# Two second-layer groups of each expert moved behind the next expert's first two first-layer groups

## The reference, cut to what matters

```
logits = x @ w_gate ; expert = argmax(logits) ; gate = softmax(logits)[expert]
for each token in order: it takes the next slot of its expert (at most 384 slots per expert)
h = relu(einsum('ecd,edf->ecf', disp, w1))        # 384 -> 1024, for each expert
y = einsum('ecf,efd->ecd', h, w2)                 # 1024 -> 384
out[token] = gate * y[expert, slot]
```

## Time and profile before

| what | value |
|---|---|
| median of 3 runs | 415.98 us (415.86 to 416.11) |
| span of the profiled execution, first to last instruction | 413.8 us |
| TensorE matmul busy | 406.2 us, 98% of the span |
| VectorE, ScalarE, GpSimd busy | 243.7, 188.1, 231.0 us |
| granted TensorE clock | full in all slices, mean 0.999 |

### The profile page before, as it was taken

How to read it: one execution, slowest core, us unless ns; L and a number is a source line. 1 busy time by engine, 2 the same in 40 slices (tenths; PEclk the granted TensorE clock), 3 DMA queues, 4 the chain that set the end, 5 groups by cost and what they waited for, 6 DMA issues and landing times.

```text
span 413.8 us, 9451 instructions
## 1 busy us (share of the span) xinstructions
PE 406.2 (98%) x3697; PEld 390.8 (94%) x3697; DVE 243.7 (59%) x576; ACT 188.1 (45%) x409; POOL 231.0 (56%) x239
## 2 busy tenths in 40 slices
PE   8999999999999999999999999999999999999994
PEld 8799799999999999999999999999999999999994
DVE  7787955376576547654653487785635556364521
ACT  4786543233433333333343555553645445464420
POOL 3789775467856685668234336075073461825531
PEclk9999999999999999999999999999999999999999
DMA  7998996204030403020018001827383845729000
GB/s 287 402 396 351 367 344 243 82 38 148 12 119 2 139 21 118 3 86 21 2 20 344 2 2 38 326 77 248 125 308 101 340 160 203 295 89 360 5 31 28
DMA packets 18650, 64.98 MB, mean 157 GB/s; under 512 B 2203, under 2 KB 11717, under 8 KB 16432
## 3 DMA queue, kind: packets, MB, share of 16 engines
q1 hardware_dynamic: 16672, 59.67, 39.5%
q0 software_dynamic: 1792, 4.73, 3.0%
q10 hardware_dynamic: 144, 0.00, 0.0%
HBM read 51.98 MB, written 13.21 MB: 158 GB/s over the span
## 4 chain that ended last, share of the span: by engine, by line
PE 92%; DVE 4%; issue 1%; POOL 1%; ACT 1%; DMA 0%; POOLq 0%; DVEq 0%
PE bank L1362 27%; PE bank L1364 26%; PE bank L1363 26%; PE bank L1383 2%; PE bank L1412 1%; PE bank L1448 1%; PE bank L1452 1%; PE bank L1686 1%; PE bank L1441 1%; PE bank L1444 1%; PE bank L1539 1%; PE bank L1721 1%; PE bank L1722 1%; PE bank L1725 1%; PE bank L1625 1%
## 5 line engine op out<-in xcount | busy, mean ns | idle before, releaser
L707 POOL TENSOR_TENSOR g_lo<-elu,g_hi 128x256 fp32r<-128x256 f32 x95 | 73.8, 778 | 86.5 <-ACT g_hi L875 86.3
L1362 PE MATMUL bank<-xt,wd_hi 128*128 128x256 f32 x285 | 80.7, 283 | 0.6 <-DVE elu L1190 0.6
L1364 PE MATMUL bank<-xt,wd_lo 128*128 128x256 f32 x285 | 80.5, 282 | 0.0
L1363 PE MATMUL bank<-xt,wd_hi 128*128 128x256 f32 x285 | 80.4, 282 | 0.0
L866 ACT ACTIVATE elu<-elu 128x256 f32<-128x256 f32 x96 | 40.1, 418 | 76.5 <-DVE elu L1182 75.9
L1362 PE MATMUL bank<-wd_hi,g_hi 128*128 128x392 f32 (+1 forms) x192 | 67.5, 352 | 0.0
L1364 PE MATMUL bank<-wd_hi,g_lo 128*128 128x392 f32 (+1 forms) x192 | 65.3, 340 | 0.0
L1363 PE MATMUL bank<-wd_lo,g_hi 128*128 128x392 f32 (+1 forms) x192 | 65.2, 339 | 0.0
L1190 DVE SCALAR_TENSOR_TENSOR elu<-elu,bank 128x256 f32<-128x256 f32 x96 | 40.3, 420 | 40.5 <-ACT elu L866 40.5
L875 ACT CAST g_hi<-elu 128x256 fp32r<-128x256 f32 x96 | 39.0, 406 | 45.0 <-DVE elu L1190 45.0
L1362 PEld LDWEIGHTS bank<-xt,wd_hi 128*128 128x128 f32 x285 | 54.0, 189 | 1.3 <-DVE elu L1190 1.1
(11 more groups left out here) (220 smaller groups left out, 946.2 us busy)
## 6 DMA issues: line engine op xcount, KB each, us to landing
we_raw<-wexp SPq DMA_DIRECT2D x8, 1536.0 KB, 6.5
wd_raw<-wexp SPq DMA_DIRECT2D x8, 1536.0 KB, 7.7
rkt<-rkt SPq DMA_DIRECT2D x12, 512.0 KB, 5.5
nat<-nat SPq DMA_DIRECT2D x9, 672.0 KB, 5.0
xrow<-slots SPq DMA_DIRECT2D x16, 193.0 KB, 7.3
wd_raw<-win SPq DMA_DIRECT2D x4, 768.0 KB, 8.0
wd_raw<-wout SPq DMA_DIRECT2D x4, 768.0 KB, 8.9
wo_tr<-wouttr SPq DMA_DIRECT2D x1, 3072.0 KB, 17.8
```

The source lines that it names most:

```text
L707: nc.gpsimd.tensor_tensor(g_lo[:, f % 4, :], elu[:, f % 2, :], g_hi[:, f % 4, :].bitcast(F32), ALU.subtract).then_inc(s_glo, 1)
L1362: mm(dst, w_hi, x_hi, start=start, stop=False)
L1363: mm(dst, w_hi, x_lo, start=False, stop=False)
L1364: return mm(dst, w_lo, x_hi, start=False, stop=stop)
```

## The change

`expert` on TensorE no longer ends with fc2(6) and fc2(7). They are issued in the next expert, fc2(6) behind its fc1(0) and fc2(7) behind its fc1(1). fc2(0) of the next expert follows fc1(2) as before. Expert 1 has nothing behind it (`behind` false, since expert 0 has another form), and expert 7 still issues all of its own. The two gate multiplications of an expert move on VectorE to behind `ge_lo` of group 1 of the next expert. Two waits are split or loosened: fc1(0) waits for one `ge_lo` less, and fc2(0) waits for the `yrow` of each tile apart. Waits on the other engines' and SyncE's side are as before.

```diff
 # VectorE
+            def expert_out(i, r):
+                for t in range(2):
+                    if t == 0:
+                        dve.wait_ge(s_y0, 2 * i + r + 1)
+                    else:
+                        dve.wait_ge(s_fc2e, ET * (2 * i + r + 1))
+                    V.tensor_scalar(yrow[r][:, t, :], ps_ye[t][:, 0:DM], xrow[r][:, t, GATE:GATE + 1], None,
+                                    ALU.mult).then_inc(s_ye[r], 1)
-            def expert(i, r, more):
+            def expert(i, r, more, behind):
                 ni, nr = (i, 1) if r == 0 else (i + 1, 0)
+                bi, br = (i - 1, 1) if r == 0 else (i, 0)
                 for f in range(ET):
...
+                    if f == 1 and behind:
+                        expert_out(bi, br)
...
+                if not more:
+                    expert_out(i, r)
 # TensorE, fc2_expert
-                    y_before, n_before = other(s_ye, r, i)
-                    wait_if(pe, y_before, 2 * n_before)
                 for t in tiles:
+                    if f == 0:
+                        y_before, n_before = other(s_ye, r, i)
+                        pe.wait_ge(y_before, 2 * n_before - 1 + t)
 # TensorE, expert
-                    wait_if(pe, s_gelo, q if f == 0 else q - 1)
+                    wait_if(pe, s_gelo, q - 1)
...
                     last.then_inc(s_he, 1)
+                    if f < 2 and behind:
+                        fc2_expert(bi, br, ET - 2 + f)
                     if more and f >= 2:
                         fc2_expert(i, r, f - 2)
...
-                if more:
-                    fc2_expert(i, r, ET - 2)
-                    fc2_expert(i, r, ET - 1)
-                else:
+                if not more:
 # both engines
-            expert(0, 1, True)
+            expert(0, 1, True, False)
...
-                expert(i, 0, True)
-                expert(i, 1, True)
-            expert(NE // 2 - 1, 0, True)
-            expert(NE // 2 - 1, 1, False)
+                expert(i, 0, True, True)
+                expert(i, 1, True, True)
+            expert(NE // 2 - 1, 0, True, True)
+            expert(NE // 2 - 1, 1, False, True)
```

More of the change, by code:

```diff
@@ L1308, in expert @@
                         V.tensor_copy(tok_i[r][:, :, :], xrow[r][:, :, TOKEN:XR]).then_inc(s_tok[r], 1)
-                for t in range(2):
-                    if t == 0:
-                        dve.wait_ge(s_y0, 2 * i + r + 1)
-                    else:
-                        dve.wait_ge(s_fc2e, ET * (2 * i + r + 1))
-                    V.tensor_scalar(yrow[r][:, t, :], ps_ye[t][:, 0:DM], xrow[r][:, t, GATE:GATE + 1], None,
-                                    ALU.mult).then_inc(s_ye[r], 1)
+                if not more:
+                    expert_out(i, r)
             tile_row(s_he, ET, s_lrow)
```

## The result

The changed kernel takes 418.35 us (median of 5 runs, 418.03 to 419.11), the kernel before 415.86 beside it: ratio 1.0069, 95% interval 1.0058 to 1.008. That is 0.7% slower, 2.5 us. The value lies inside the stated range, but it isn't the forecast of 416.0: it is where rival 1 (the loads are late in full, 418.3 to 419.7, chance 0.36) put it. The profiled execution has a span of 417.0 us, 3.2 above the one before; at 418.82 us it was one of the longer of the five.

What follows compares the result with a forecast made beforehand. TensorE, busy 98% of the span, was taken as the bound. From 415.98 us, -0.94 for the removed gap and +1.0 for late rows gave 416.0 us, own range 415.2 to 416.8; full range 414.9 to 419.2.

Steps and rivals of the forecast that it cites:

- rival 1: SyncE's loads late in full, no overlap of fetch and pause helping: net +2.4 to +3.7, 418.3 to 419.7 us, chance 0.36.
- The gain: TensorE at fc1(2): the wait for fc1(0)'s bank goes in six of seven places, 6 x 0.156 = 0.94 us.
- The place of the loss: SyncE's queue: W2 issued 5.21 and rows 6.1 us behind W1, transposes waiting for late rows, 1.0 us (0.2 to 1.7).
- The `yrow` multiplications: VectorE's two gate multiplications, moved behind `ge_lo`: both tiles ready for fc2(0) in time by 0.4 us, cost nothing.
- the signs of being wrong: In the changed profile: transposes idle 1 us and more, or none; fc2(0)'s weight load idle; fetches not 5 to 7 us behind W1.
- So the rows land 0.9 to 1.4 us later.: SyncE's row loads behind W2: landing shift; experts 5 and 6 in time or late by 0.1, before any fetch effect.
- the pause of W2 issued alone: DMA engines after a lone W2 issue: full flow only 2.3 us behind it, 1.4 us of flow lost.
- a fetch there costs the loads much less: Instruction fetches of experts 3, 4, 7 fall where little flows, 5.6 to 7.5 us behind W1: rows late by 0 to 0.5.
- the 415.0: Time if W2 loads at the skill's price, landing 0.5 us earlier: no row late, sum -0.94.
- GpSimd's 0.11 us: fc2(0)'s wait for W2's three low parts: margin falls from 0.27 to 0.11 us ahead of the weight load, should just hold.
- rival 3: At fc2(0), the gap only moved to a wait for GpSimd or `yrow`: net 0 on its own, counted inside the forecast's 0.40.
- Nothing there: GpSimd's scatter of `yrow`, queued behind the W2 pieces until 306.23: `yrow` at 305.95 still ahead, so no cost.

Runs made afterwards that it cites:

- both waits out of the way: Changed kernel with row loads issued ahead of W1 and fc2(0), fc2(2), fc2(5) each waiting only for its GpSimd W2 piece: 414.75 us; old order with early rows 415.79.
- experiment 4: Changed kernel, but fc2(0), fc2(2) and fc2(5) wait for GpSimd's first, second and third W2 piece: 418.65 us, ratio 1.0065.
- the half move: Against the changed kernel, fc2(6) stays in its expert, only fc2(7) goes behind the next fc1(0), gate multiplications behind `ge_lo` of group 0: 421.8 us, ratio 1.0157.
- experiment 1: Kernel before, TensorE's order untouched, SyncE holding W2 of experts 3 to 7 until the next expert's fc1(1): 418.04 us, ratio 1.0051.
- the kernels with the rows ahead of W1: Gates copied aside on VectorE, row loads issued before W1: changed kernel 415.48 us, kernel before 415.79; with finer W2 waits, full change 414.75, fc2(7) alone moved 414.69.
- experiment 3: Changed kernel with SyncE's last two loads exchanged, rows first, then W2: 417.89 us, ratio 1.0044.

## Why the prediction was right and wrong

**What held.** The gain: the gap at fc1(2) is gone in six places, and with both waits out of the way the move gives about 1.0 us (415.79 to 414.75), against 0.94. The place of the loss: W2 and rows out at 5.2 and 6.1, the transposes late, all five. The `yrow` multiplications are in time (nothing at fc2(0) is left once GpSimd's wait is finer). VectorE's other work cost nothing.

**How much of that is luck.** The range holds 418.35 because it was drawn round the rivals too. The forecast's own 416.0, with 415.2 to 416.8, missed it by 2.35 us, and a slower kernel had a chance of 0.36 only. The time lies at the lower end of rival 1. Two of the signs of being wrong that the prediction names did show: idle of 1 us and more at the transposes (1.03 and 1.32), and a late weight load at fc2(0).

**What failed.** The forecast fell on one step: "So the rows land 0.9 to 1.4 us later." For experts 5 and 6, whose loads had no instruction fetch of 0.02 MB in them, it was 2.1 and 2.0, and TensorE idled 0.85 and 0.34 us for them instead of 0 to 0.1. The other three places, which the forecast built on these two, idled 3.0 us together instead of 0.9. I took the pause of W2 issued alone and let everything behind it run at the old rate. The windows show that the rate itself falls, to 266 GB/s over 6 us, and that the pause is the smaller part of it. The term was 1.4 us at most, and measured 1.9 to 2.1. The lower bound of 0.9 rests on a W2 that lands 6.1 us behind its issue, as a W1 does, though the row of the W2 issued alone says 8.0; measured were 6.4 to 7.5.

**The fetch.** Experts 3, 4 and 7, with a fetch among their packets, were shifted by 1.1, 0.6 and 1.0 us only, so the difference between them and 5 and 6 fell from about 1.6 us to 0.4. That is what the step "a fetch there costs the loads much less" said. It is consistent with it and not shown: no run was made to move a fetch. In one run of experiment 4 (the finer wait alone) expert 7's fetch lay 0.9 us behind W1 instead of 5.1, and its rows landed at 14.1 instead of 14.5; expert 3's, with the fetch where it was, differ more between the same two runs (14.2 and 15.1), so this doesn't decide it. Rival 1 got the time right for a partly wrong reason: its price rested on three late places with 5 and 6 in time; measured were five late ones, each by about 0.3 to 1.3.

**The price of a transfer.** W2 took 6.4 to 7.5 us when issued at 5.24 in the changed kernel and 8.6 to 9.8 at 4.18 in the half move. The Trainium skill, in DMA: Bandwidth & Descriptors (Anatomy of one DMA), fits a transfer issued by GpSimd with 2.0 us and the rest at 436 GB/s, which would be an estimate of 5.6 us. These loads are issued by SyncE, for which that section gives no fit, and no W2 here was that fast, so the 415.0 that would follow from it didn't come.

**GpSimd's 0.11 us** of margin did not hold. I had taken 0.04 us for the semaphore, from a VectorE row; from GpSimd's end (324.67) to the weight load (324.91) it is 0.24. That is rival 3, 0.3 to 0.4 us, counted inside the forecast. In the changed kernel it cost nothing that can be told (418.35 us with it, 418.65 with the finer wait), because the late rows come behind it.

**The scatter.** "Nothing there" did not hold either. The prediction set the first `yrow` tile, 305.95, against the end of GpSimd's pieces, but the scatter starts behind both tiles:

```profile
306.85 0.99 POOL L729 DMA_INDIRECT out<-yrow,tok_i  x1 [0.60 <-DVE yrow L1295]
```

GpSimd waits 0.5 to 0.6 us there for each expert. No time is seen lost by it: the late loads with the scatter in its old place (experiment 1) landed the rows at nearly the same distances.

## What to carry to other kernels

Where an order on the busiest engine is changed, list what hangs on each moved instruction's semaphore, above all the loads; the engine's own gap is seldom the largest number. Take small transfers off the end of such a chain (a copy of 128x2 elements lets the rows go out 1.3 us ahead of W1 instead of 3.8 behind it, or 6.1 with the changed order), and let each use wait for the piece that it needs. Then the same order that lost 2.5 us wins 1.1. And a gap that is closed ahead of a late transfer gives nothing: the engine only arrives at the wait sooner.

## What the runs showed of the hardware that wasn't expected

A second transfer of 1.5 MB on one queue did not land the earlier the earlier it was issued. Where the rows follow it on the queue, W2 landed 9.8 to 12.2 us behind the first's issue when issued at 3.1, 12.4 to 14.2 at 4.2, and 11.6 to 13.1 at 5.2 (one of 15 at 14.0). The 4.2 was the worst with TensorE's old and new order alike. Both late starts lower the flow over expert 5's 6 us window, from 394 to between 266 and 280 GB/s, and in each run the DMA share falls far less (0.96 or 0.97 to between 0.82 and 0.86). In the kernels with the rows ahead of W1 no transposes waited, and the order differed: 13.0 to 13.4 at 4.2, 12.9 to 15.0 at 5.25. Why a late start lowers the flow, and whether the DMA engines fall out of step with each other, stays open: no run isolates it. Each of these landings is from one profiled execution of its kernel.

A wait for GpSimd's last piece let the weight load start 0.24 us behind the end of that piece as the profile has it, a wait for VectorE's 0.04 us behind; ends on GpSimd are rough, but in experiment 3 it was 0.25 from such an end (361.39) to the matmul behind it.
